# Five unread matmuls in place of two, unread products on 32-byte multiples, and one minimum for two tiles

## What is computed

```python
batch, n_heads, seq, head_dim = (4, 8, 576, 64)
scores = scale * np.matmul(q, k.transpose(0, 1, 3, 2))
kth = np.partition(scores, -top_k, axis=-1)[..., -top_k:-top_k + 1]   # top_k = 32
mask = scores >= kth
scores = np.where(mask, scores, -1000000000.0)
scores = scores - np.max(scores, axis=-1, keepdims=True)
attn = np.exp(scores)
attn = attn / (np.sum(attn, axis=-1, keepdims=True) + 1e-09)
return np.matmul(attn, v)
```

## Time and profile before

| | us |
|---|---|
| median of 3 runs | 1120.54 (1118.74 to 1121.85) |
| the profiled execution, its own time | 1121.11 |
| its span, first to last instruction | 1119.3 |
| time around the span | 1.8 |
| mean granted clock of PE over the span | 0.933 |
| attention, from the start to about | 670 |

### The profile page before, as it was taken

One profiled execution on the slowest core, in us unless ns is written; L12 is line 12 of the kernel. 1 busy time (PEld: TensorE's weight loads), 2 busy tenths in 40 slices (PEclk: granted clock), 3 DMA queues, 4 the chain that ended last, 5 costly groups with the idle time before them and its releaser, 6 DMA issues.

```text
span 1119.3 us, 20476 instructions
## 1 busy us (share of the span) xinstructions
PE 914.5 (82%) x5825; PEld 642.2 (57%) x5825; DVE 815.9 (73%) x1870; ACT 620.8 (55%) x1199; POOL 707.6 (63%) x900
## 2 busy tenths in 40 slices
PE   3887887788788788888777888965789999999995
PEld 1555555555555555555555566312477877788884
DVE  5899999999999999999999993107535424444331
ACT  5787877877877878777777762002414312331110
POOL 2788898988888889888888881002124434444443
PEclk9999999989989999989999989977889999999998
DMA  9910110011011011011011004899814434433332
GB/s 354 381 44 1 46 45 20 23 44 44 0 44 44 0 44 44 0 44 44 0 44 44 0 0 167 326 422 422 369 22 105 70 86 115 109 44 40 39 42 31
DMA packets 21584, 105.11 MB, mean 94 GB/s; under 512 B 2944, under 2 KB 4016, under 8 KB 12464
## 3 DMA queue, kind: packets, MB, share of 16 engines
q1 hardware_dynamic: 13696, 84.54, 19.2%
q0 software_dynamic: 7136, 11.20, 7.6%
q10 hardware_dynamic: 720, 8.98, 2.2%
HBM read 88.37 MB, written 16.07 MB: 93 GB/s over the span
## 4 chain that ended last, share of the span: by engine, by line
PE 41%; DVE 32%; issue 18%; DMA 4%; ACT 2%; DVEq 1%; POOL 1%; SPq 0%; ACTq 0%; POOLq 0%
PE psum L803 12%; PE psum L562 9%; DVE arena L994 8%; DVE arena L1001 5%; PE psum L808 5%; PE psum L521 4%; DVE arena L990 3%; DVE arena L986 3%; DVE arena L978 2%; DVE arena L1007 2%; DMA arena<-w_soft 2%; PE psum L792 2%; PE psum L533 2%; DMA arena<-xs_rows,arena 2%; DVE arena L982 2%
## 5 line engine op out<-in xcount | busy, mean ns | idle before, releaser
L1287 POOL TENSOR_SCALAR arena<-arena 128x576 bf16<-128x576 f32 x142 | 246.8, 1738 | 66.8 <-issue 32.9
L562 PE MATMUL psum<-arena 128*128 128x130 f32 (+3 forms) x1600 | 256.5, 307 | 0.2 <-ACT arena L853 0.2
L562 PEld LDWEIGHTS psum<-arena 128*128 128x128 f32 (+3 forms) x1600 | 214.3, 202 | 46.0 <-issue 12.1
L521 PE MATMUL psum<-arena 64*128 64x288 f32 (+1 forms) x640 | 117.8, 473 | 136.8 <-DVE arena L986 131.3
L1296 POOL TENSOR_TENSOR arena<-arena 128x576 f32<-128x576 f32 x142 | 178.5, 1277 | 0.0
L958 ACT ACTIVATE h_hi<-psum 128x512 fp32r<-128x512 f32 x80 | 43.6, 596 | 214.3 <-PE psum L792 214.3
L834 ACT ACTIVATE arena<-psum,arena 128x576 bf16<-128x576 f32 x144 | 106.6, 740 | 84.5 <-DVE arena L978 84.3
L521 PEld LDWEIGHTS psum<-arena 64*128 64x128 f32 (+1 forms) x640 | 46.4, 180 | 182.8 <-DVE arena L986 153.7
L1235 DVE COPY arena<-psum 128x512 f32 x41 | 28.4, 692 | 163.5 <-PE psum L808 147.8
L803 PE MATMUL psum<-w_hi,h_hi 128*128 128x512 f32 x320 | 133.5, 417 | 5.6 <-DVE arena L1235 2.8
L803 PE MATMUL psum<-w_lo,h_hi 128*128 128x512 f32 x320 | 128.1, 400 | 0.0
(11 more groups left out here) (192 smaller groups left out, 1529.5 us busy)
## 6 DMA issues: line engine op xcount, KB each, us to landing
weights<-w_soft SPq DMA_DIRECT2D x21, 1024.0 KB, 16.4
arena<-qkv SPq DMA_DIRECT2D x15, 1189.0 KB, 5.2
weights<-w_top SPq DMA_DIRECT2D x12, 1024.0 KB, 27.3
arena<-w_soft SPq DMA_DIRECT2D x11, 1024.0 KB, 12.4
weights<-w_top SPq DMA_DIRECT2D x3, 2048.0 KB, 20.0
weights<-w_top ACTq DMA_DIRECT2D x3, 2048.0 KB, 7.6
out<-arena SPq DMA_DIRECT2D x1, 4864.0 KB, 17.6
arena<-w_top SPq DMA_DIRECT2D x4, 1024.0 KB, 27.6
```

The costliest lines, as they stand in the source:

```text
L521: last = nc.tensor.matmul(bank(2 * (t % 2) + x, SH)[q0:q0 + rows, :], qT[u][half, w * P + q0:w * P + q0 + rows], kT[u][half, h * SH:(h + 1 ...
L562: last = nc.tensor.matmul(o_place(n, k)[0:rows, :], wT[0:kr, t % 2, kc, q0:q0 + rows], v_, start=(kc == 0), stop=(kc == KC - 1))
L1287: nc.gpsimd.tensor_scalar(keep[t % 2], s_sb[t % S_SLOTS], kth_sb[:, t % S_SLOTS:t % S_SLOTS + 1], None, ALU.is_ge) \
```

## The change

Three edits.

1. `keep_warm` issues five of its matmuls in place of two, in each duo in which it issued two.
2. The 25 unread products of `select` of tile a go to float 1 of `list_f`, which is a multiple of 32 bytes, and those of tile b to float 33, a multiple as well. Before, tile a's stood at float 0, which is none, and tile b's at float 25, which is one.
3. The minimum of `n_hit` and 32 is taken once for both tiles of a duo, over two neighbouring columns, at the place where tile a's stood. Tile b's is gone. `select` waits for the count of duos instead of that of tiles; both `n_hit` were written by then, since L982 of b, ahead of it on DVE, waits for `strike` of b, and that for the marks of b.

```diff
+WARM = 5
...
+        list_at = at[0] - 2 * COLS
...
-        chosen = [list_f[:, a * PICKED:(a + 1) * PICKED] for a in range(2)]
+        chosen = [list_f[:, a:a + PICKED] for a in (-list_at % 8, -list_at % 8 + TOPK)]
...
                 pe.wait_ge(o_copied, DPI * j + n + 1 + 1)
-                for _ in range(2):
+                for _ in range(WARM):
                     nc.tensor.matmul(bank(7), strike_w, cst[:, 0:BANK // 2].bitcast(BF16), start=True, stop=True,
...
             def fourth8(j, n, x, t):
-                slot = t % S_SLOTS
-                nc.vector.tensor_scalar(n_sat[:, slot:slot + 1], n_hit[:, slot:slot + 1], float(TOPK), None,
-                                        ALU.min).then_inc(saturated, 1)
+                if x == 0:
+                    slot = t % S_SLOTS
+                    nc.vector.tensor_scalar(n_sat[:, slot:slot + 2], n_hit[:, slot:slot + 2], float(TOPK), None,
+                                            ALU.min).then_inc(saturated, 1)
                 hold(dve, struck24, TPI * j + t + 1)
                 nc.vector.max(top(t, 3), work[t % 2]).then_inc(top32, 1)
...
-                dve.wait_ge(saturated, TPI * j + t + 1)
+                dve.wait_ge(saturated, DPI * j + n + 1)
```

## The result

The changed kernel takes **1136.95 us** (median of 4 runs, 1129.48 to 1143.72) where the kernel before takes 1119.78 (median of 4, 1118.74 to 1121.85): **1.0149 times as long, 95% interval 1.0076 to 1.0223**. It is slower; the forecast was 1115 in a range of 1096 to 1122. Its runs also lie further apart, 14 us against 3; the profiled execution took 1133.14 with a span of 1131.3, 12.0 more than the span before.

What follows compares the result with a forecast made beforehand. Attention was taken as bound by DVE's own work plus falls of the clock; from 1121.1 us, -17.2 - 1 + 0 - 4.3 + 16.1 + 0.5 = -5.9 gave 1115.2, stated as 1115, range 1096 to 1122.

Steps and rivals of the forecast that it cites:

- The clock: Pause ahead of `qk` of tile a: five unread matmuls fill it, all clock falls in attention go, -17.2 us.
- The place: `select` of tile a: moving its unread products to a 32-byte multiple gains nothing, 0 us (ends -0.5 and +0.5).
- Tile b's minimum gone: DVE in attention: dropping this minimum saves 0.06 us in each of 72, -4.3 us.
- The wide minimum waits for POOL's first operation: DVE beside POOL's first L1296: two columns are held until it ends, net +0.24 us in 67 duos, +16.1 us.
- the third rival: The minimum is held through both of POOL's L1296, 1.24 us longer each time: +83, about 1198 us; chance 0.04.
- The rival of the clock: Pause ahead of `qk` of a: the clock keeps falling, the 17.2 us don't come, 1127 us; chance 0.13.

Runs made afterwards that it cites:

- edit 1 alone: Five unread matmuls in place of two, everything else as in the kernel before: 0.9849 of the kernel before, 1104.16 us.
- minimum early: The changed kernel with the two-column minimum moved ahead of `second8` of tile b, where POOL is idle: 0.9824 of the kernel before, 1100.98 us.
- POOL earlier: The changed kernel with POOL's two small operations for the negated maxima made one: 0.9911 of the kernel before, 1109.54 us.
- edit 3 alone: The changed kernel with two unread matmuls and the unread products at their old place: 1.0370 of the kernel before, 1161.90 us.

## Why the prediction was wrong, step by step

**The clock.** Right in kind: filling the pause takes the falls away, and where the pause has 1.0 to 1.25 us there are none. Its size was 13.5 in place of 17.2, since I priced the duos by the ordinary one and left 0.6 for three late ones, and there are fifteen. In the trace of before POOL is late in ten duos; two of them stand there without a fall, at 8.99 and 9.07, and the other eight have a fall, where their 0.28 us don't show.

**The place.** Right: nothing, [0.9981, 1.0012].

**Tile b's minimum gone.** Right in size: 8.81 (edit 1 alone) to 8.75 (minimum early) is the 0.06 per duo. The proof is not clean, since the place of what is left changed too, and with two narrow minimums in the other place a duo is 8.75 as well.

**The wide minimum waits for POOL's first operation.** Right, in its mechanism and in size: 0.505 us, the end some 0.03 after that of POOL's operation, `select` of a at 0.22, a pause of 1.20 (1.25 forecast), a duo of 8.955 (8.99). Against 8.75 without the wait that is 0.205 us, where I had 0.24. With the double wait away (POOL earlier), the kernel took 1109.54, 0.9911, on the forecast's side and inside its range; some 3 of the 5 us below 1115 lie ahead of the 67 duos, where I had priced 0.5 more and not less.

**The step that failed** is the dismissal of the third rival, "the minimum waits for both of POOL's L1296". I priced it for all duos at once (+83) and gave it 0.04 by a single row: a select that got in behind the first of three L1317 at 324.92. Neither half holds. The rival isn't all or nothing: it is there in 11 of the 67 duos and costs 15.6 us, and another 7.5 in the five falls behind it. This stretch takes 15.9 us more in place of 5.1 less (-17.2 - 4.0 + 16.1), 21.0 in all; these 23.1 are the whole of it, and the ordinary duo, cheaper than forecast, gives some 2 back. And a row on three small operations says nothing on two of 128x576; no row of before has a held operation that came in the first of such a pair; `select` of a, where it met the pair in attention, always came in the second. I had written that no row shows an operation of two columns, but not that no row shows one that meets the first of such a pair and is held. I took the nearest row for a reason that excludes, and 0.04 for what no row of this kind shows was too little.

Could the trace of before have told? The condition stands in it: of its masks of tile b in the 67 duos ten start 0.38 to 0.44 us after the readout and at once behind L1317. One of them comes right behind the very `select` that I cited (325.20 to 325.63). From the timeline of before:

```profile
325.12 0.08 DVE L1007 DVE_READ_ACCUMULATOR arena<-arena 128x1 f32 x1
...
325.63 1.73 POOL L1287 TENSOR_SCALAR arena<-arena 128x576 bf16<-128x576 f32 x1
```

That these are the duos in which a held operation would wait twice, it doesn't tell.

**The rival of the clock** stated that a longer pause gives a part of the fill back. That is what happens behind the eleven duos, five times, though by another cause.

The Trainium skill, in "SBUF — State Buffer", Who interferes with whom, has the loser of the shared ports blocked for the whole of the other's instruction. The ordinary duo agrees, with 0.50 us. In the eleven others it was blocked for 1.93 us and two instructions, which that sentence alone doesn't give; here the measurement decides.

## What to carry to other kernels

Merging small VectorE operations on SBUF can cost more than it saves: beside a busy GpSimd, two of one column (0.06 us each, start to start) were cheaper than one of two columns, which took 0.42 or 1.83. If a wide one is needed, put it where GpSimd has no long operation, and look for the duos in which GpSimd never waits, since there one wait becomes several. Filling TensorE's pause with unread matmuls paid: with three in each duo in place of two the falls in attention were 2 in place of 21, and with five there were none. And it is the late duos (two of nine here) that have to be looked up in the trace before an ordinary duo is multiplied.

## What the runs showed of the hardware that I had not expected

- GpSimd can keep a VectorE operation out over two and three of its instructions in a row (1.93 and up to 2.94 us). In 36 of 36 such cases GpSimd had come to the first of three 128x576 operations with its semaphore already there (0.38 us or more after the signalling instruction's end); in 53 of 53 where it came to it without a pause too, but started 0.18 to 0.21 us after that end, the operation got in after one. The condition was found by sorting; why it makes a difference stays open.
- At 1.64 us of pause ahead of `qk` the clock fell in 21 of 67 duos and at 1.43 in 2 of 67; at 1.85, with edit 3 alone, in 36. That five of the eleven pauses of 2.45 us brought a fall and six did not is not explained.
- The wide minimum costs about the same by two ways: with two unread matmuls 3.7%, some 26 of 37 us by falls, and with five 3.0% (1.0149 over 0.9849), half of it by double waits.
- The changed kernel's runs spread over 14 us and those of edit 3 alone over 12, where all others spread over 8 or less. Whether another number of duos with the double wait or of falls stands behind this, one profiled execution of each can't show.
